# Gate and value of an MLP by seven block products for eight

## What is computed

```python
def _moe2_ref(x, w_gate, w_val, w_out, rms_g):     # x: 1152 tokens x 512; w_gate, w_val: 512 x 1536
    rms = np.sqrt(np.mean(x * x, axis=-1, keepdims=True) + 1e-06)
    xn = x / rms * rms_g
    g = xn @ w_gate
    silu = g * (1.0 / (1.0 + np.exp(-g)))
    val = xn @ w_val
    return (silu * val @ w_out).astype(np.float32)
```

## Time and profile before

| | |
|---|---|
| median of 3 runs | 679.21 us (678.59 to 681.27) |
| span of the profiled execution | 677.1 us |
| mean granted TensorE clock | 1.000 of full speed |
| TensorE busy | 667.8 us, 99% |
| DVE, ACT, GpSimd busy | 75%, 64%, 66% |
| gaps of TensorE | none shown between 390 and 660 us |

### The profile page before, as it was taken

How to read it: one execution, slowest core, us unless ns; L and a number is a source line. 1 busy time by engine, 2 the same in 40 slices (tenths; PEclk the granted TensorE clock), 3 DMA queues, 4 the chain that set the end, 5 groups by cost and what they waited for, 6 DMA issues and landing times.

```text
span 677.1 us, 12086 instructions
## 1 busy us (share of the span) xinstructions
PE 667.8 (99%) x3956; PEld 624.6 (92%) x3956; DVE 509.7 (75%) x1002; ACT 430.9 (64%) x1005; POOL 447.0 (66%) x452
## 2 busy tenths in 40 slices
PE   7899999999999999999999999999999999999998
PEld 5899999999999999998899999899999999999997
DVE  6899999999999958987889889967554444444433
ACT  5888989899898988988888888843511111111110
POOL 6887999999999979999989789760566540000000
PEclk9999999999999999999999999999999999999999
DMA  7657467665746320101110110111121210000012
GB/s 230 198 161 208 127 179 229 182 186 165 203 137 167 103 89 0 47 18 62 63 63 1 64 63 10 53 63 63 52 73 63 70 55 1 1 0 1 1 58 83
DMA packets 26157, 60.77 MB, mean 90 GB/s; under 512 B 3320, under 2 KB 8192, under 8 KB 25984
## 3 DMA queue, kind: packets, MB, share of 16 engines
q1 hardware_dynamic: 25824, 59.87, 29.1%
q10 hardware_dynamic: 288, 0.33, 0.2%
HBM read 43.78 MB, written 2.40 MB: 68 GB/s over the span
## 4 chain that ended last, share of the span: by engine, by line
PE 84%; POOL 11%; DMA 2%; issue 1%; DVE 1%; ACT 0%; SPq 0%; POOLq 0%; ACTq 0%; DVEq 0%
PE hb L948 28%; PE ob L1016 20%; PE sc L855 11%; PE sc L865 10%; PE pv_ps L883 6%; PE misc L883 5%; POOL num L806 3%; POOL num L808 3%; PE tb L948 2%; POOL wi_lo L719 1%; POOL wo_lo L719 1%; POOL wi_hi L717 1%; DMA wraw<-in_moe_w_out 1%; DMA qrawA<-in_q 1%; DMA wraw<-in_moe_w_in 1%
## 5 line engine op out<-in xcount | busy, mean ns | idle before, releaser
L1270 DVE TENSOR_REDUCE neg_part<-sc 128x1 f32<-128x384 f32 x216 | 106.8, 548 | 9.5 <-PE sc L855 8.0
L1279 DVE TENSOR_TENSOR pt_lo<-sc,pt_hi 128x384 fp32r<-128x384 f32 x216 | 107.5, 549 | 2.2 <-ACT pt_hi L1094 1.3
L1094 ACT ACTIVATE pt_hi<-sc 128x384 fp32r<-128x384 f32 x216 | 92.8, 494 | 24.8 <-PE sc L865 20.9
L1085 ACT ACTIVATE prob<-sc,neg_max 128x768 f32<-128x768 f32 (+1 forms) x144 | 106.2, 757 | 2.7 <-DVE neg_max L1272 2.7
L1016 PE MATMUL ob<-wo_hi,gt_hi 128*128 128x512 f32 x248 | 97.7, 394 | 1.3 <-DVE tok L1374 0.8
L1016 PE MATMUL ob<-wo_hi,gt_lo 128*128 128x512 f32 x248 | 97.3, 392 | 0.0
L1016 PE MATMUL ob<-wo_lo,gt_hi 128*128 128x512 f32 x248 | 96.5, 389 | 0.0
L948 PE MATMUL hb<-xt_hi,wi_hi 128*128 128x384 f32 x280 | 94.6, 338 | 0.0
L948 PE MATMUL hb<-xt_lo,wi_hi 128*128 128x384 f32 x280 | 94.1, 336 | 0.0
L948 PE MATMUL hb<-xt_hi,wi_lo 128*128 128x384 f32 x280 | 93.9, 335 | 0.0
L865 PE MATMUL sc<-ident,prob 128*128 128x128 f32 x648 | 82.4, 272 | 0.0
(11 more groups left out here) (184 smaller groups left out, 1732.3 us busy)
## 6 DMA issues: line engine op xcount, KB each, us to landing
wraw<-in_moe_w_out SPq DMA_DIRECT2D x6, 1024.0 KB, 5.0
krawB<-in_k SPq DMA_DIRECT2D x8, 576.0 KB, 4.3
qrawB<-in_q SPq DMA_DIRECT2D x8, 512.0 KB, 5.2
krawA<-in_k SPq DMA_DIRECT2D x7, 576.0 KB, 4.4
o_part<-o_sb SPq DMA_DIRECT2D x14, 288.0 KB, 3.7
qrawA<-in_q SPq DMA_DIRECT2D x7, 512.0 KB, 5.2
wraw<-in_moe_w_in SPq DMA_DIRECT2D x3, 1024.0 KB, 6.4
wraw<-in_moe_w_gate SPq DMA_DIRECT2D x3, 1024.0 KB, 5.1
```

Source lines behind the costliest of these rows:

```text
L1085: nc.scalar.activation(dst, sc[s][:, c0:c1, 0:KBANK], ACT.Exp, bias=neg_max[:, s:s + 1], accum_out=sum_parts[:, (s + i) % 2, i, part:part ...
L1094: nc.scalar.activation(pt[0][:, 3 * c:3 * c + 3, PT_COL[i]:PT_COL[i] + P], src, ACT.Copy).then_inc(pt_hi, 1)
L1270: nc.vector.tensor_reduce(neg_part[:, s, c:c + 1], sc[s][:, c, 0:KBANK], AX.X, ALU.max, negate=True).then_inc(part_done, 1)
L1279: nc.vector.tensor_tensor(pt[1][:, kt, col], src, pt[0][:, kt, col].bitcast(F32), ALU.subtract).then_inc(pt_lo, 1)
```

## The change

Gate and value of one channel block are written as a product of 2 x 2 blocks: the weights are (gate, value) by (lower, upper half of the depth of 512), the tokens are (lower, upper half of the depth) by (first, second 64 of each tile). Seven products of such blocks, some of sums of blocks, replace eight. A11, A12 are the halves of gate, A22 the upper half of value; S1 to S4 are sums of weight blocks. B11, B21, B22 are token blocks, T1 to T4 sums of token blocks. GpSimd forms the S sums and splits all seven weight blocks of a channel block (`weights_plain`, `weights_sums`, `weights_last`, `weights_hi`, `weights_lo`): scalar forms of 512, 256 and 1024 columns and tensor-tensor operations of 512, five times 256, and 1024 columns, into one of three slots. DVE forms the T sums.

Tokens are in two parts: tiles 0 to 3 (256 columns of 64 per tile) and 4 to 8 (320 columns). A *group* is one channel block for one part: seven products of six matmuls, in four banks. There are 24, in the order f0, f1, f2 of part 0, the same of part 1, and then each block with both parts. In the banks the results need additions: U2 = P6 + P1, U3 = P7 + U2, upper value = P5 + U3, upper gate = P3 (added by TensorE on top of what P5 left) + U2, lower value = P4 + U3, lower gate = P1 + P2 (by TensorE). ACT copies P1 out of its bank first (`first_copy`).

A token tile now goes: transposes, four scalings of 128 columns out of the bank into `turned` (ACT), four sums of 128 columns (DVE), high parts of 256, 128 and 512 columns (ACT), low parts of the same (DVE). `turned` has two buffers. The factor 1/rms goes to gate only before the silu, and for value it is in the final accumulation. Raw weights come block by block (256 KB) into a ring of four; the output weights of the second MLP have one split buffer instead of two, and GpSimd does channel block 0 between the last units of the first MLP.

The new order of TensorE at the hand-over, first before and then in the changed kernel (its own line numbers; names in brackets are semaphores; L1016 and L1240 are outer products, L942 and L1141 transposes of tokens, L934 and L1133 those of the scales, L948 and L1180 products of gate and value).

The diff, cut to what sets order and waits:

```diff
+PART_TILES = ((0, SPLIT), (SPLIT, TILES))
...
+GROUPS2 = [(f, part) for part in range(2) for f in range(SLOTS)]
+GROUPS2 += [(f, part) for f in range(SLOTS, 12) for part in range(2)]
...
+        def outs_behind(g):
+            f, part = GROUPS2[g]
+            c, k = divmod(f, CHUNK)
+            if part == 1 and k == CHUNK - 1:
+                return [(c, t) for t in range(SPLIT if c < NC2 - 1 else TILES - 1)]
+            if part == 0 and k == 0 and c > 0:
+                return [(c - 1, t) for t in range(SPLIT, TILES)]
+            return []
...
+                if i < RAWS:
+                    sp.wait_ge(w_split, 8 * len(order))
+                elif RAW2[i - RAWS][0] == "o":
+                    sp.wait_ge(o_split, 2 * RAW2[i - RAWS][1] + 2)
+                else:
+                    sp.wait_ge(f_split, F_OPS * RAW2[i - RAWS][1] + F_FREE)
...
+                if f == 0:
+                    pool.wait_ge(s1_done, UNITS * (NC1 - 1))
+                elif f == 1:
+                    pool.wait_ge(s1_done, UNITS * NC1)
+                elif f == 2:
+                    pool.wait_ge(g_full, UNITS * NC1)
+                else:
+                    pool.wait_ge(p3_done, group_at(f - SLOTS, 1) + 1)
...
+                if f % CHUNK == 0:
+                    pool.wait_ge(s2_done, TILES * (NC1 + f // CHUNK))
...
+            first_weights = {4: weights_plain, 5: weights_sums, 6: weights_last, 7: weights_hi, 9: weights_lo}
...
+            weights_plain(1)
             newton_root(0)
+            weights_sums(1)
+            weights_last(1)
+            weights_hi(1)
+            weights_lo(1)
+            weights_plain(2)
+            weights_sums(2)
+            weights_last(2)
             newton_root(1)
+            weights_hi(2)
+            weights_lo(2)
+            for unit, f in UNITS2[3:]:
+                if unit == "o":
+                    split_o(f)
...
+            def group(g):
+                f, part = GROUPS2[g]
+                n, w, x = PART_COLS[part], slots[f % SLOTS], xw[part]
+                def block_product(bank, a, b, first, last):
+                    for d in range(2):
+                        for k, (i, j) in enumerate(((0, 0), (1, 0), (0, 1))):
+                            ins = nc.tensor.matmul(bank[:, 0:n], w[i][:, a, d], x[j][:, b, d], start=first and d == 0 and k == 0,
+                                                   stop=last and d == 1 and k == 2, skip_group_check=True)
+                    return ins
+                if part == 0:
+                    pe.wait_ge(f_split, F_OPS * f + F_OPS)
+                pe.wait_ge(xw_lo, 3 * PART_TILES[part][1])
+                if g == 0:
+                    pe.wait_ge(g_lo, UNITS * NC1)
                 else:
+                    pe.wait_ge(gate_low, g)
+                block_product(bank_a, A11, B11, True, True).then_inc(p1_done, 1)
+                if g > 0:
+                    pe.wait_ge(val_low, g)
+                block_product(bank_x, S2, T2, True, True).then_inc(p6_done, 1)
+                block_product(bank_y, S3, T3, True, True).then_inc(p7_done, 1)
+                if g > 0:
+                    pe.wait_ge(gate_sum, g)
+                block_product(bank_z, S1, T1, True, True).then_inc(p5_done, 1)
+                pe.wait_ge(p1_copied, g + 1)
+                block_product(bank_a, A12, B21, False, True).then_inc(p2_done, 1)
+                pe.wait_ge(u2_done, g + 1)
+                block_product(bank_x, A22, T4, True, True).then_inc(p4_done, 1)
+                pe.wait_ge(val_high, g + 1)
+                block_product(bank_z, S4, B22, False, True).then_inc(p3_done, 1)
...
+            second_product(NC1 - 1, 3)
+            second_product(NC1 - 1, 4)
+            turn_tokens(2)
+            second_product(NC1 - 1, 5)
+            turn_tokens(3)
+            second_product(NC1 - 1, 6)
+            turn_scales(0)
+            second_product(NC1 - 1, 7)
+            turn_tokens(4)
+            second_product(NC1 - 1, 8)
+            turn_tokens(5)
+            group(0)
+            turn_tokens(6)
+            group(1)
+            turn_tokens(7)
+            turn_tokens(8)
+            group(2)
+            turn_scales(1)
+            turn_scales(2)
+            for g in range(SLOTS, len(GROUPS2)):
+                group(g)
+                for c, t in outs_behind(g):
+                    second_product(NC1 + c, t)
...
+            def tokens_scale(t):
+                act.wait_ge(xt_t, t + 1)
+                if t >= 2:
+                    act.wait_ge(xw_lo, 3 * t - 3)
+                for d in range(DK):
...
+            def first_copy(g):
+                n = PART_COLS[GROUPS2[g][1]]
+                act.wait_ge(p1_done, g + 1)
+                if g >= 2:
+                    act.wait_ge(gate_sum, g - 1)
+                nc.scalar.activation(sums_p[g % 2][:, 0:n], bank_a[:, 0:n], ACT.Copy).then_inc(p1_copied, 1)
...
+            def tokens_sums(t):
+                part, col = place(t)
+                x, full = turned[t % 2], xw_full[part]
+                x11, x21, x12, x22 = (x[:, d:d + 2, c:c + HALF_TILE] for c in (0, HALF_TILE) for d in (0, 2))
+                dve.wait_ge(xt_scaled, DK * t + DK)
+                nc.vector.tensor_tensor(full[:, T1, :, col], x12, x11, ALU.subtract).then_inc(t_full, 1)
+                nc.vector.tensor_tensor(full[:, T3, :, col], x22, x12, ALU.subtract).then_inc(t_full, 1)
+                dve.wait_ge(t_full, 4 * t + 1)
+                nc.vector.tensor_tensor(full[:, T2, :, col], x22, full[:, T1, :, col], ALU.subtract).then_inc(t_full, 1)
+                dve.wait_ge(t_full, 4 * t + 3)
+                nc.vector.tensor_tensor(full[:, T4, :, col], x21, full[:, T2, :, col], ALU.subtract).then_inc(t_full, 1)
...
+            def sums_start(g):
...
+                dve.wait_ge(p6_done, g + 1)
+                dve.wait_ge(p1_copied, g + 1)
+                nc.vector.tensor_tensor(u2[:, 0:n], bank_x[:, 0:n], u2[:, 0:n], ALU.add).then_inc(u2_done, 1)
+                dve.wait_ge(p7_done, g + 1)
+                dve.wait_ge(u2_done, g + 1)
+                nc.vector.tensor_tensor(u3[:, 0:n], bank_y[:, 0:n], u2[:, 0:n], ALU.add).then_inc(u3_done, 1)
+            def value_high(g):
...
+                dve.wait_ge(p5_done, g + 1)
...
+                dve.wait_ge(u3_done, g + 1)
+                if g > 0:
+                    dve.wait_ge(act_full, g)
+                nc.vector.tensor_tensor(val[:, 1, 0:n], bank_z[:, 0:n], third_sum[:, 0:n], ALU.add).then_inc(val_high, 1)
...
+                dve.wait_ge(p4_done, g + 1)
+                nc.vector.tensor_tensor(val[:, 0, 0:n], bank_x[:, 0:n], third_sum[:, 0:n], ALU.add).then_inc(val_low, 1)
+                dve.wait_ge(p3_done, g + 1)
+                nc.vector.tensor_tensor(y, bank_z[:, 0:n], sums_p[g % 2][:, 0:n], ALU.add).then_inc(gate_sum, 1)
+                dve.wait_ge(gate_sum, g + 1)
+                nc.vector.tensor_tensor(by_tiles(y), by_tiles(y), scales_of(part, 1), ALU.mult).then_inc(gate_high, 1)
...
+            for g in range(SLOTS, len(GROUPS2)):
+                late = g > SLOTS and not outs_behind(g - 1)
+                sums_start(g)
+                if late:
+                    act_product(g - 1)
+                value_high(g)
+                gate_low_part(g)
+                if late:
+                    act_lo_part(g - 1)
+                sums_end(g)
+                for j, (c, t) in enumerate(outs_behind(g)):
+                    accumulate2(c, t)
+                    if j == 0:
+                        act_product(g)
+                    if j == 1:
+                        act_lo_part(g)
```

More of the change, by code:

```diff
@@ L321, in build @@
             order += [("in", c), ("out", c)]
-        for c in range(NC2):
-            order += [("gate", c), ("val", c), ("out2", c)]
         at = {key: j for j, key in enumerate(order)}
@@ new lines, in tokens_hi @@
+            def tokens_hi(t):
+                part, x = t // SPLIT if t < TILES - 1 else 1, turned[t % 2]
+                hi, full = xw[part][0], xw_full[part]
+                c0 = HALF_TILE * (t - PART_TILES[part][0])
+                col = slice(c0, c0 + HALF_TILE)
+                act.wait_ge(xt_scaled, DK * t + DK)
+                nc.scalar.activation(hi[:, B11:B22].rearrange("p j d n -> p (j d) n")[:, :, col], x[:, :, 0:HALF_TILE], ACT.Copy).then_inc(xw_hi, 1)
+                nc.scalar.activation(hi[:, B22, :, col], x[:, 2:4, HALF_TILE:P], ACT.Copy).then_inc(xw_hi, 1)
+                act.wait_ge(t_full, 4 * t + 4)
+                nc.scalar.activation(hi[:, T1:].rearrange("p j d n -> p (j d) n")[:, :, col],
+                                     full[:, T1:].rearrange("p j d n -> p (j d) n")[:, :, col], ACT.Copy).then_inc(xw_hi, 1)
@@ new lines, in first_copy, with silu @@
+            def first_copy(g):
[4 more added lines that the diff above has]
+                nc.scalar.activation(sums_p[g % 2][:, 0:n], bank_a[:, 0:n], ACT.Copy).then_inc(p1_copied, 1)
+            def silu(g):
```

(67 more changed lines are left out.)

488 lines of the change are left out of this document (287 added, 201 removed).

## The result

The changed kernel takes **712.91 us** (median of 4 runs, 712.48 to 715.34), the kernel before 678.9 in the runs beside it: 1.050 times as long, 95% interval 1.049 to 1.052. I had forecast 691, range 669 to 702. The direction was right, the size was not: 22 us are missing. The span of the profiled execution is 710.7 us.

What follows compares the result with a forecast made beforehand. TensorE, busy 99%, was taken to bound the kernel. Span: 677.1 - 16.7 (products) + 6.6 (hand-over) + 12.2 (groups 0 to 2) + 6 (collisions) + 4 (later groups) = 689.2; time 691 us, range 669 to 702.

Steps and rivals of the forecast that it cites:

- TensorE's part: Gate and value products: 150.0 us become 133.3 with matmuls every 0.1178 and 0.1467 us, a gain of 16.7 us.
- VectorE's prices: DVE operations: 0.20, 0.33, 0.40 and 0.73 us at 128, 256, 320 and 640 columns; 128 and 640 lie outside the rows.
- rival 2: Whole kernel: no stall at all, if 128-column SBUF operations are far cheaper than the line; 662.5 us, chance 0.05.
- The schedule up to 443: Hand-over start, scheduled by hand: TensorE waits 2.4 us for an accumulation, then 2.3 for g_lo of unit 47.
- Groups 0 to 2: First three groups, carrying tiles 4 to 8: 28.9 us for 16.7 without a gap, so 12.2 us lost.
- Cost between 0 and 18; I take 6: Hand-over: DVE's two-SBUF token operations collide with GpSimd's 17 tensor-tensors (18 us); 6 us taken, half of DVE's waits being for ACT.
- The price of 0.4 each, from `den`: First MLP's two-SBUF operation `den` beside busy GpSimd takes 0.99 us in the mean: about 0.4 more per operation.
- Rival 4: Hand-over: the DVE-GpSimd lock decides, costing 18 us for 6 once they alternate one for one; 703 us, chance 0.08.
- Nothing for most groups, 0.2 on average: 4 us: Groups 3 to 23: collisions with GpSimd mostly hidden by slack; 4 us lost in all, bounds 0 and 17.
- The slack of 0.8, and of 0.3 to 0.4: Groups 3 to 23: time DVE's operations have before TensorE waits, 0.8 us at 320 columns, 0.3 to 0.4 at 256.
- The clock: After TensorE's gaps: products at a lower granted clock, listed as a sign of being wrong, with no size given.
- Rival 5: Second MLP: GpSimd late with weights, TensorE waiting 3 us at each of three places; 9 more, 700 us, chance 0.09.

Runs made afterwards that it cites:

- q_all: Changed kernel with GpSimd's splits and sums left out for channel blocks 1 to 11 and all output weights, for measuring only: 686.1 us, ratio 1.012.
- pieces: Changed kernel with GpSimd's operations for channel blocks and output weights cut into pieces of at most 256 columns: 711.0 us, ratio 1.047.
- q_hand: Changed kernel with GpSimd's work for channel blocks 1 and 2 and output weights 0 to 2 replaced by constant writes: 702.0 us, ratio 1.034.

## Why the prediction was wrong

- **TensorE's part** (16.7 us gained): right. Matmuls come at the forecast distance, and with GpSimd quiet the rest is 195.8 us.
- **VectorE's prices** outside the rows: right. Without GpSimd a 128-column operation lasts 0.28 us, and the next starts 0.20 behind it, as the line gave; that closes rival 2.
- **The schedule up to 443**: right. Waits of 2.05 and 2.00 for 2.4 and 2.3; without collisions group 0 starts 17.7 us after (3,5), for 16.8.
- **Groups 0 to 2** (28.9 us): too kind by 3.4. I followed P1's copy, but not the turns of tiles 7 and 8, which stand behind group 1. The rest of the 4.3 is 0.9 ahead of group 0.
- **"Cost between 0 and 18; I take 6"**: the step that failed first. It is 14.1. The mechanism was right, its size was not. My reason, that half of DVE's waits there are for ACT, counts idle time of DVE, which collisions do not need: the 63 operations of the nine tiles lost 15.2 us, about as much as the hand-over lost by them. The price of 0.4 each, from `den`, was not too low (15.2/63 = 0.24); what failed is the discount from 18 to 6 for time that I thought hidden. Nor does the loss go by DVE's columns (0.42 in the mean for the second sum of a tile, of 128, and 0.12 for the low part of 512); in the lines shown it is what is left of GpSimd's instruction, and I had just made the operations many and small. Rival 4 named that mechanism and its price; with a chance of 0.08 it was far too low.
- **"Nothing for most groups, 0.2 on average: 4 us"**: the second. It is 12.9. In the 21 groups the three two-SBUF operations lose 27 us by their means (12 x (0.69 + 0.31 + 0.23) + 9 x (0.35 + 0.72 + 0.34), each the mean of the changed kernel less that of q_all), some 1.3 us a group and 0.43 an operation, so the price of 0.4 held. The slack of 0.8, and of 0.3 to 0.4, did not cover it: I had counted each place alone against its slack, when all three stand in one string on DVE, and TensorE waited at the value's sums behind them. From the first matmul of one group to that of the next, against q_all, 9.9 of the 12.9 us fall in six groups (5, 6, 7, 11, 15 and 19), 1.1 to 2.2 each; "nothing" was right for a third of the groups only. The upper bound of 17 held.
- **The clock**: named as a sign of being wrong, not priced. 2 us.
- **Rival 5**: not in the changed kernel, but 9.2 us of it in `pieces`, so the margin was thin.

The errors, 8.1 + 8.9 + 4.3, are 21 of the 22 us; the clock, at full again from 503 us on, is within the first and third. What stays open is how the 14.1 divides into the waits themselves and the lower clock that they bring.

The Trainium skill (SBUF — State Buffer, Who interferes with whom) also says that a GpSimd instruction that only writes SBUF leaves a two-SBUF VectorE instruction alone. The trace of q_hand agrees: GpSimd wrote constants with this memset,

```profile
443.35 1.60 POOL L930 MEMSET slot_hi<- 128x1792 f32 x1
```

and DVE's low part beside it took 0.42 us:

```profile
443.43 0.42 DVE L1691 TENSOR_TENSOR x_lo<-turned,x_hi 128x256 fp32r<-128x256 f32 x1
```

In the changed kernel, beside a subtraction, it took 1.50.

## What to carry to other kernels

Before many small two-SBUF operations are given to VectorE, see what GpSimd does then: each can wait for a whole GpSimd instruction (0.28 us became 2.50), so count operations and GpSimd's durations, not columns. One operand in PSUM removed it at nearly the same price, where a bank was free; shorter GpSimd instructions lessened it, but help only while GpSimd has time to spare. And fewer TensorE columns are worth nothing where the helpers' added work makes the hand-over longer than that: here a saving of 16.7 stood against 15.6 us lost at the hand-over even without collisions and in the better order.
